# A gated scan and an ELU feed-forward on one core: the side work of the first block spread thinner, the weight sums of pairs 4 to 7 made and split in the second block

## What is computed

```python
sig = 1 / (1 + exp(-f_logit))                      # [2, 6080, 256]
f = lower_bound + (1 - lower_bound) * sig
h[t] = f[t] * h[t-1] + (1 - f[t]) * x[t]           # scan over the sequence
a = h.reshape(12160, 256)
g = elu(a @ w_in)                                  # w_in [256, 2048]
out = g @ w_out                                    # w_out [2048, 256]
```

## Time and profile before

| | |
|---|---|
| median of 3 runs | 961.97 us (961.41 to 965.41) |
| profiled execution | 961.75 us |
| its span, first to last instruction | 959.9 us |
| PE busy | 954.5 us, 99% |
| ACT, DVE, POOL busy | 82%, 75%, 66% |
| granted clock of TensorE | 1.000 |

### The profile page before, as it was taken

How to read it: one execution, slowest core, us unless ns; L and a number is a source line. 1 busy time by engine, 2 the same in 40 slices (tenths; PEclk the granted TensorE clock), 3 DMA queues, 4 the chain that set the end, 5 groups by cost and what they waited for, 6 DMA issues and landing times.

```text
span 959.9 us, 15015 instructions
## 1 busy us (share of the span) xinstructions
PE 954.5 (99%) x4362; PEld 815.6 (85%) x4362; DVE 722.9 (75%) x916; ACT 790.1 (82%) x1424; POOL 628.8 (66%) x475
## 2 busy tenths in 40 slices
PE   9999999999999999999999999999999999999998
PEld 6999888888888888888888888888888888888887
DVE  6998976976886796697688679678768867966444
ACT  7989888878888888888888888888888788887775
POOL 2588796576667668557656755856775765676544
PEclk9999999999999999999999999999999999999999
DMA  7212012002102201100210210120021021001001
GB/s 273 68 33 95 1 33 66 34 1 78 55 1 57 76 1 44 55 33 2 74 55 0 66 66 0 46 66 18 23 65 44 0 76 55 0 0 46 1 1 45
DMA packets 23078, 42.02 MB, mean 44 GB/s; under 512 B 2560, under 2 KB 4096, under 8 KB 23040
## 3 DMA queue, kind: packets, MB, share of 16 engines
q1 hardware_dynamic: 22752, 41.10, 13.2%
q10 hardware_dynamic: 288, 0.46, 0.2%
HBM read 29.10 MB, written 12.45 MB: 43 GB/s over the span
## 4 chain that ended last, share of the span: by engine, by line
PE 95%; ACT 2%; DVE 1%; issue 0%; DMA 0%; ACTq 0%; DVEq 0%
PE acc L893 17%; PE acc L895 17%; PE acc L894 17%; PE h L863 14%; PE h L865 14%; PE h L864 14%; ACT e L469 1%; PE h L998 1%; PE h L1000 1%; PE h L999 1%; ACT e L463 1%; DMA opening<-first_gate 0%; DVE x L625 0%; ACT opening L419 0%; PE h L964 0%
## 5 line engine op out<-in xcount | busy, mean ns | idle before, releaser
L335 POOL TENSOR_TENSOR g_lo<-e,g_hi 128x512 fp32r<-128x512 f32 (+1 forms) x384 | 516.6, 1356 | 325.2 <-ACT g_hi L477 323.8
L463 ACT ACTIVATE e<-h 128x512 f32<-128x512 f32 (+1 forms) x379 | 224.9, 594 | 124.3 <-PE h L865 90.1
L716 DVE SCALAR_TENSOR_TENSOR e<-e,h 128x512 f32<-128x512 f32 (+1 forms) x379 | 256.8, 677 | 70.2 <-ACT e L469 69.0
L893 PE MATMUL acc<-g_hi,w_out_hi 128*128 128x512 f32 (+1 forms) x768 | 291.1, 379 | 0.4 <-DVE w_out_lo L687 0.4
L895 PE MATMUL acc<-g_hi,w_out_lo 128*128 128x512 f32 (+1 forms) x768 | 291.0, 379 | 0.0
L894 PE MATMUL acc<-g_lo,w_out_hi 128*128 128x512 f32 (+1 forms) x768 | 290.9, 379 | 0.0
L469 ACT ACTIVATE e<-e 128x512 f32<-128x512 f32 (+1 forms) x384 | 241.2, 628 | 9.6 <-issue 1.1
L477 ACT CAST g_hi<-e 128x512 fp32r<-128x512 f32 (+1 forms) x384 | 232.0, 604 | 19.4 <-DVE e L716 19.4
L863 PE MATMUL h<-a_hi,w_in_hi 128*128 128x512 f32 x616 | 234.7, 381 | 0.0
L865 PE MATMUL h<-a_hi,w_in_lo 128*128 128x512 f32 x616 | 234.7, 381 | 0.0
L864 PE MATMUL h<-a_lo,w_in_hi 128*128 128x512 f32 x616 | 234.7, 381 | 0.0
(11 more groups left out here) (75 smaller groups left out, 555.8 us busy)
## 6 DMA issues: line engine op xcount, KB each, us to landing
opening<-forget_logit SPq DMA_DIRECT2D x44, 256.0 KB, 2.6
x<-value SPq DMA_DIRECT2D x44, 256.0 KB, 2.7
out<-out_sb SPq DMA_DIRECT2D x44, 256.0 KB, 2.0
w_in_raw<-w_in SPq DMA_DIRECT2D x8, 256.0 KB, 5.5
w_out_raw<-w_out SPq DMA_DIRECT2D x8, 256.0 KB, 6.6
out<-out_sb SPq DMA_DIRECT2D x4, 224.0 KB, 2.1
x<-value SPq DMA_DIRECT2D x3, 224.0 KB, 6.3
opening<-forget_logit SPq DMA_DIRECT2D x2, 224.0 KB, 6.4
```

The lines of the kernel that those rows point to most:

```text
L335: nc.gpsimd.tensor_tensor(g_lo[:, t % RING, 0:w], e[:, t % TILES, 0:w], g_hi[:, t % RING, 0:w].bitcast(F32), ALU.subtract).then_inc(g_lo_r ...
L463: nc.scalar.activation(e[:, i, 0:w], bank_of(j, t)[:, 0:w], ACT.Relu, scale=-1.0).then_inc(r_ready, 1)
L716: nc.vector.scalar_tensor_tensor(e[:, t % TILES, 0:w], e[:, t % TILES, 0:w], -1.0, bank_of(j, t)[:, 0:w], ALU.add, ALU.max).then_inc(g_rea ...
L893: nc.tensor.matmul(bank, hi, g_h, start=opens, stop=False)
```

## The change

In the first block the side work behind a tile is at most one scan or two short operations on VectorE, and mostly one on ScalarE. The gate work of block 1 (`tanh`, `open_gate`, `weigh`, `scan`) comes 3 to 4 tiles later, from tile 12 to 22; `combine` is done in two tiles, two at a time; w_out of pair 6 is rounded and split after tiles 11 and 12 in place of 12 and 14, w_out of pair 7 after 24 and 28 in place of 18 and 25.

The weight sums of pairs 4 to 7 leave the first block. VectorE makes them in block 1, in pairs 0 and 1, two adds of four pairs' width each, between the `elu` of C12 and that of C22. ScalarE rounds them in pairs 2 to 5 of block 1 (before: in a row after tile 30, and the last piece after tile 31's product). GpSimd splits those of pairs 4 and 5 in pairs 2 and 3 of block 1 (before: 0 and 1), those of 6 and 7 in pairs 3 to 5 about as before, and the first three columns of pair 3's in pair 0 of block 1, not after tile 27.

```diff
--- before.py
+++ after.py
@@ -324,7 +324,7 @@
                 if begin < P5:
                     pool.wait_ge(w_sums_ready, PAIRS // 2 * 4 * (p // (PAIRS // 2) + 1))
                 else:
-                    pool.wait_ge(w_in_hi_ready, p + 1 if p < PAIRS - 1 else PAIRS + 1)
+                    pool.wait_ge(w_in_hi_ready, p + 1)
                 nc.gpsimd.tensor_tensor(w_in_lo[:, p, begin:end], w_in_raw[:, p, begin:end],
                                         w_in_hi[:, p, begin:end].bitcast(F32),
                                         ALU.subtract).then_inc(w_in_lo_ready[p], end - begin)
@@ -377,10 +377,10 @@
             def second_spare(q, i):
 
                 at = (q, i)
-                if at in ((0, C22), (1, C12), (3, C22), (4, C21)):
-                    w_in_rest({(0, C22): 4, (1, C12): 5, (3, C22): 6, (4, C21): 7}[at], P1, P5)
-                if at in ((0, C11), (0, C12), (1, C11), (1, C22), (4, C12), (5, C12)):
-                    w_in_rest({(0, C11): 2, (0, C12): 3, (1, C11): 4, (1, C22): 5, (4, C12): 6, (5, C12): 7}[at],
+                if at in ((0, C22), (2, C12), (2, C21), (3, C21), (4, C21)):
+                    w_in_rest({(0, C22): 3, (2, C12): 4, (2, C21): 5, (3, C21): 6, (4, C21): 7}[at], P1, P5)
+                if at in ((0, C11), (0, C12), (2, C22), (3, C22), (4, C12), (5, C12)):
+                    w_in_rest({(0, C11): 2, (0, C12): 3, (2, C22): 4, (3, C22): 5, (4, C12): 6, (5, C12): 7}[at],
                               P5, PRODUCTS)
 
             def whole(j, par, last=False):
@@ -393,10 +393,10 @@
             nc.gpsimd.memset(a_hi[:, 0, P5, SHORT:TILE].bitcast(F32), 0.0).then_inc(zeros_ready, 1)
             for t in range(TILES * PAIRS):
                 rest_g(0, t)
-                if t in (18, 21):
-                    rest(1, 1, {18: P1, 21: P2}[t])
-                if t in (25, 27):
-                    w_in_rest({25: 2, 27: 3}[t], P1, P5)
+                if t in (22, 24):
+                    rest(1, 1, {22: P1, 24: P2}[t])
+                if t == 26:
+                    w_in_rest(2, P1, P5)
                 if t == 30:
                     rest(1, 1, P4)
             for q in range(PAIRS):
@@ -484,18 +484,12 @@
                 act.wait_ge(w_in_loaded[p], 16)
                 nc.scalar.copy(w_in_hi[:, p, 0:4], w_in_raw[:, p, 0:4]).then_inc(w_plain_hi_ready, 1)
 
-            def round_sums(p, begin=P5):
+            def round_sums(p):
 
                 act.wait_ge(w_sums_ready, PAIRS // 2 * 4 * (p // (PAIRS // 2) + 1))
-                if begin == P5:
-                    q, i = divmod(plain_done(p) - 1, TILES)
-                    act.wait_ge(done_of[i], q + 1)
-                nc.scalar.copy(w_in_hi[:, p, begin:], w_in_raw[:, p, begin:]).then_inc(w_in_hi_ready, 1)
-
-            def round_last_sum():
-                p = PAIRS - 1
-                act.wait_ge(c21_ready, PAIRS)
-                nc.scalar.copy(w_in_hi[:, p, P5], w_in_raw[:, p, P5]).then_inc(w_in_hi_ready, 1)
+                q, i = divmod(plain_done(p) - 1, TILES)
+                act.wait_ge(done_of[i], q + 1)
+                nc.scalar.copy(w_in_hi[:, p, P5:], w_in_raw[:, p, P5:]).then_inc(w_in_hi_ready, 1)
 
             def round_w_out(p):
                 act.wait_ge(w_out_loaded[p], 16)
@@ -524,32 +518,33 @@
                     split(j + 1, 1 - par, {6: P6, 7: P3}[q])
 
             def first_spare(t):
-                if t in (0, 2, 3, 6, 13):
-                    round_plain({0: 3, 2: 4, 3: 5, 6: 6, 13: 7}[t])
-                if t in (1, 4, 7, 8, 10, 12, 18):
-                    round_w_out({1: 1, 4: 2, 7: 3, 8: 4, 10: 5, 12: 6, 18: 7}[t])
+                if t in (0, 2, 3, 6, 14):
+                    round_plain({0: 3, 2: 4, 3: 5, 6: 6, 14: 7}[t])
+                if t in (1, 4, 7, 8, 10, 11, 24):
+                    round_w_out({1: 1, 4: 2, 7: 3, 8: 4, 10: 5, 11: 6, 24: 7}[t])
                 if t in (4, 5):
                     tanh(0, 1, t - 4)
                 if t in (7, 9):
                     split_first(1, t // 9)
                 if t in (8, 11):
                     keep_carry(0, t // 11)
-                if t in (9, 11, 13, 15):
-                    tanh(1, t // 13, {9: 0, 11: 1, 13: 0, 15: 1}[t])
-                if t in (10, 12, 14, 16):
-                    open_gate(1, t // 14, {10: 0, 12: 1, 14: 0, 16: 1}[t])
-                if t in (16, 20):
-                    keep_carry(1, t // 20)
-                if t in (14, 16, 22, 23, 24, 25):
-                    split(1, 1, {14: P1, 16: P2, 22: P5, 23: P6, 24: P7, 25: P3}[t])
-                if t in (18, 19, 28, 29):
-                    round_sums({18: 0, 19: 1, 28: 2, 29: 3}[t])
-                if t == 30:
-                    for p in range(PAIRS // 2, PAIRS - 1):
-                        round_sums(p)
-                    round_sums(PAIRS - 1, P6)
-
-            def whole(j, par, last=False):
+                if t in (12, 15, 17, 19):
+                    tanh(1, t // 17, {12: 0, 15: 1, 17: 0, 19: 1}[t])
+                if t in (13, 16, 18, 20):
+                    open_gate(1, t // 18, {13: 0, 16: 1, 18: 0, 20: 1}[t])
+                if t in (19, 24):
+                    keep_carry(1, t // 24)
+                if t in (21, 22, 24, 25, 26, 27):
+                    split(1, 1, {21: P1, 22: P2, 24: P5, 25: P6, 26: P7, 27: P3}[t])
+                if t in (23, 25, 28, 29):
+                    round_sums({23: 0, 25: 1, 28: 2, 29: 3}[t])
+
+            def second_spare(q):
+
+                if q in (2, 3, 4, 5):
+                    round_sums(q + 2)
+
+            def whole(j, par, last=False, second=False):
                 for q in range(PAIRS):
                     t = TILES * q
                     negative(*before(j, q, C21))
@@ -561,6 +556,8 @@
                     exp(j, t + C11)
                     round_g(*before(j, q, C21))
                     late(j, par, q, last)
+                    if second:
+                        second_spare(q)
                     round_g(j, t + C11)
                     negative(j, t + C12)
                     exp(j, t + C12)
@@ -588,8 +585,7 @@
                     round_g(0, t - 1)
                 exp(0, t)
                 first_spare(t)
-            round_last_sum()
-            whole(1, 1)
+            whole(1, 1, second=True)
             whole(2, 0)
             with nc.Fori(1, (BLOCKS - 2) // 2, engines=(mybir.EngineType.Activation,),
                          hint_back_edge=True) as i:
@@ -776,10 +772,10 @@
                     rest(n, other, P3)
 
             def first_spare(t):
-                if t in (0, 2, 3, 6, 15):
-                    w_plain_rest({0: 3, 2: 4, 3: 5, 6: 6, 15: 7}[t])
-                if t in (1, 4, 7, 9, 10, 14, 25):
-                    w_out_rest({1: 1, 4: 2, 7: 3, 9: 4, 10: 5, 14: 6, 25: 7}[t])
+                if t in (0, 2, 3, 6, 16):
+                    w_plain_rest({0: 3, 2: 4, 3: 5, 6: 6, 16: 7}[t])
+                if t in (1, 4, 7, 9, 10, 12, 28):
+                    w_out_rest({1: 1, 4: 2, 7: 3, 9: 4, 10: 5, 12: 6, 28: 7}[t])
                 if t in (4, 5):
                     open_gate(0, 1, t - 4)
                 if t in (5, 7):
@@ -788,22 +784,27 @@
                     scan(0, 1, t // 8)
                 if t in (8, 9):
                     rest(0, 0, (P5, P4)[t - 8])
-                if t in (11, 13, 16, 18):
-                    weigh(1, t // 16, {11: 0, 13: 1, 16: 0, 18: 1}[t])
-                if t in (12, 14, 17, 19):
-                    scan(1, t // 17, {12: 0, 14: 1, 17: 0, 19: 1}[t])
-                if t in (20, 21, 22, 23):
-                    combine(1, t - 20)
-                if t in (10, 11, 13, 15):
-                    w_sum(0, PAIRS // 2, {10: 0, 11: 1, 13: 2, 15: 3}[t])
-                if t in (16, 18, 20, 24):
-                    w_sum(PAIRS // 2, PAIRS // 2, {16: 0, 18: 1, 20: 2, 24: 3}[t])
-                if t in (22, 27):
+                if t in (14, 17, 19, 21):
+                    weigh(1, t // 19, {14: 0, 17: 1, 19: 0, 21: 1}[t])
+                if t in (15, 18, 20, 22):
+                    scan(1, t // 20, {15: 0, 18: 1, 20: 0, 22: 1}[t])
+                if t in (23, 24):
+                    combine(1, 2 * (t - 23))
+                    combine(1, 2 * (t - 23) + 1)
+                if t in (11, 13, 14, 16):
+                    w_sum(0, PAIRS // 2, {11: 0, 13: 1, 14: 2, 16: 3}[t])
+                if t in (25, 27):
                     w_in_rest(t // 27)
-                if t in (28, 29, 30):
-                    rest(1, 1, (P5, P6, P3)[t - 28])
-
-            def whole(j, par, last=False):
+                if t in (26, 28, 29, 30):
+                    rest(1, 1, {26: P5, 28: P6, 29: P7, 30: P3}[t])
+
+            def second_spare(q, place):
+
+                if place == 3 and q in (0, 1):
+                    w_sum(PAIRS // 2, PAIRS // 2, 2 * q)
+                    w_sum(PAIRS // 2, PAIRS // 2, 2 * q + 1)
+
+            def whole(j, par, last=False, second=False):
```

(5 more changed lines are left out.)

## The result

The changed kernel takes 1000.94 us (1000.08 to 1001.95, 5 runs) against 961.55 (5 runs): ratio 1.040, 95% interval 1.039 to 1.042. The prediction said 961.2.

A forecast was written before the change was run, and what follows sets the result against it. PE's matmuls were taken to bound the kernel, with only 1.9 us of first-block waits to win. Those waits go and pair 0's second sum loses to GpSimd: -1.9 + 1.3 = -0.6, so 961.2, range 959.4 to 963.2.

The forecast's parts named there:

- The bound on the gain: First block, from 16.12 us to the first 512-wide product: PE loses 1.9 us, the most the change can win.
- the bank waits: First block, from tile 20 on: PE waits for PSUM banks freed by VectorE's late `elu`; predicted gone with 1.6 us to spare.
- 1.3 us lost: Second block, pair 1: product P2, due at 91.24, waits for `fork` and starts at about 92.55.
- case 4: Second block, pairs 0 and 1: GpSimd gets in ahead of each sum; 3.0 us lost against 1.9 won, 962.9; chance 0.10.
- case 5: Pairs 2 to 5: GpSimd so late that PE waits for `w_in_lo`; 2 to 5 us, 963 to 966; chance 0.02.
- slow restarts: First block: PE restarting slowly behind waits; together with the PSUM bank waits, the other 1.1 us lost.
- the cost is nothing: Second block: moved ScalarE roundings and GpSimd splits cost nothing, unless GpSimd's queue runs over 3.5 us late.
- 4 us of cover: Second block: GpSimd splits the weights of pairs 4 and 5 at least 4 us before PE wants them.
- The named risk: Second block, pair 0: the second sum loses to GpSimd's subtraction, delaying `fork` and P2 of pair 1 by 1.3 us; chance 0.48.
- what breaks GpSimd's row: Second block, pair 0: VectorE's gate opening at 85.78 breaks GpSimd's row of two, which could start at 84.83.
- case 2: Second block: the second sum of pair 0 gets in, or `fork`'s delay hides; 1.9 us stay won, 959.9; chance 0.28.

## Why the prediction was wrong

**The bound on the gain: right.** It said 1.9 us could be won in the first block and the first wide product would start near 77.6. It started at 77.65, with no wait between 16 us and there. VectorE's split of w_out for pair 6 came at 39.2 (44.88 in the earlier trace rows) where I had said near 39, and the bank waits were gone.

**The step that failed: what a stall costs.** The prediction priced a stall at its length ("1.3 us lost"), and had case 4 as the dearest likely one, 962.9. All its prices of late work are of that kind. Here a stall also decides the pace of all matmuls behind it: one load late by 0.04 us cost 40.8 us. The sentence "only case 5 or something unseen could lose it" left this at 0.02. In the trace of before every late load lay in the first block, among 448-column matmuls, so none shows a lasting loss. One sign was there: behind the stall at 66.5 us six steps took 0.199 to 0.216 us in place of 0.193, at a granted clock of 1.00, before the pace was back at 68.1. The prediction booked this with the "slow restarts" and did not ask whether it would end among 512-column matmuls; whether it is the same slow pace is not shown. The rare runs of before near 1004 have the length that the second pace would give, but none of them has a profile, and none was among the three times that the prediction had.

**The second step: "the cost is nothing" for GpSimd's splits.** I asked only whether GpSimd keeps its own deadlines (4 us of cover), and it did. But the two engines hold each other up: work added to GpSimd makes VectorE's instructions late. That was in the earlier trace rows, and I had used it for the sums alone. `weigh` in pair 3 took 1.50 us in place of 0.68, which is 0.82 more; `add_u4` had some 0.78 us of room, and missed by 0.04.

**The named risk was real but smaller.** `fork` behind the two sums and P2 behind `fork` came late by 0.12 us in one run and in time in another; I had 1.3 us. In the profile both sums ran uncovered (0.68 and 0.69 us): GpSimd had held VectorE up one step earlier, at the gate opening (1.53 us), which pushed `add_c22` and the `elu` of C12 until GpSimd's split was over. I had counted that opening only as what breaks GpSimd's row and had given it no delay of its own, and its late `add_c22` held up P4 by 0.13. So the two sums got in, as in case 2, and the way to it was another. The size for `fork` was wrong by ten times, and even the small size is enough.

**What stays open.** Why the interleaved order has two paces, and what decides whether a late load changes the pace. In the profiled runs in that order, sixteen late loads behind 80 us met the fast pace (one right behind another counted once). Eleven were followed by the slow one (late by 0.04 to 2.4 us); five left it alone (0.03 us at 112.5 and 0.04 at 884.9 in the run with nine narrow matmuls, 0.05 at 142.1, 0.12 at 86.05, 0.42 at 112.4). So the size alone doesn't decide. No trace shows the fast pace lost behind 80 us without a late load. Open too is why narrow matmuls end the slow pace in some cases (89.2 in the changed kernel, the nine at 158) and not in others (89.5 with the sums moved alone, 88 in the run with nine wide ones).

## What to carry to other kernels

When TensorE is full, count the matmuls of a window or take the distance between their starts; PE's busy share and the clock stayed at 99% and 1.00 here while the pace fell by 5%. Ask of a change not only how long PE might wait but whether it waits at all, and check each weight load against the matmul before it. Work put on GpSimd was here also a delay for the VectorE instructions beside it, those with two SBUF inputs and the gate opening with one, so price it in VectorE's queue, at the places where PE's next product hangs on that queue.

## What the runs showed of the hardware

With the columns interleaved as here, 512-column float32r matmuls with a weight load each follow each other at 0.2200 or at 0.2307 us, at a granted clock of 1.00, and hold either for hundreds of microseconds; in plain order at 0.2267 in both runs made. A load late by 0.04, 0.27 or 2.4 us brought the same slow pace, and one late by 0.42 did not. A second late load brought the fast one back in one run (125.7 us) and not in another (125.9 us, in the run with nine narrow matmuls). Nine 448-column matmuls brought it back in the profiled run, and nine of 512 did not. The Trainium skill, "TensorE: Matmul & The Clock Gate", section "Back-to-back issue gap", gives the gap of a matmul by itself as N / 2.4 + 2.5 ns, some 216 ns for 512 columns, and about 131 ns for 512 columns in a sustained stream of weight loads and matmuls; none of the three paces measured here is either.

A VectorE gate opening (128x512, one SBUF input) takes 0.54 us alone and took 1.53 while GpSimd subtracted; `weigh` (two inputs) took 0.68 and up to 1.78.
